# Blocked delta-rule attention before two MoE layers: products taken 22 groups ahead instead of 20, and a queue of transfers put in another order

## The reference

```python
k_n = k / (norm(k) + 1e-06)
for t in range(S):
    y[:, :, t] = einsum('bhd,bhde->bhe', q[:, :, t], state)
    v_old = einsum('bhde,bhd->bhe', state, kt)
    state = state + bt * einsum('bhd,bhe->bhde', kt, vt - v_old)
x = attention_out                    # 3072 tokens x 384
h = x @ w_in;  g = P(h) / (Q(h) + 1e-06);  x = g @ w_out      # first layer
h = x @ w_in;  g = relu(h) ** 2;           out = g @ w_out    # second layer
```

## Time and profile before

| what | us |
|---|---|
| median of three runs (1150.89 to 1154.31) | 1152.41 |
| the profiled execution | 1150.53 |
| its span, first to last instruction | 1148.8 |
| attention: start_z(0) at, last matmul at | 53.1, 339 |
| first matmul of the MoE layers at | 345.1 |

### The profile page before, as it was taken

How to read it: one execution, slowest core, us unless ns; L and a number is a source line. 1 busy time by engine, 2 the same in 40 slices (tenths; PEclk the granted TensorE clock), 3 DMA queues, 4 the chain that set the end, 5 groups by cost and what they waited for, 6 DMA issues and landing times.

```text
span 1148.8 us, 18205 instructions
## 1 busy us (share of the span) xinstructions
PE 1101.6 (96%) x6352; PEld 950.1 (83%) x6352; DVE 674.8 (59%) x1110; ACT 656.2 (57%) x1315; POOL 509.5 (44%) x634
## 2 busy tenths in 40 slices
PE   8798989999878999999999999899999999999998
PEld 6598989999876878888888888788888888888886
DVE  6984445533228988888887878865343333434332
ACT  5665656744448968787777878745333333333332
POOL 5186884877006887777777877600000000000000
PEclk9998989999997999999999999999999999999999
DMA  9937676663504101010100103150010101010000
GB/s 192 205 68 183 125 153 142 112 127 75 152 22 151 42 1 55 1 55 1 56 1 1 56 1 111 42 151 29 20 36 1 55 1 55 1 55 1 1 29 28
DMA packets 173627, 74.42 MB, mean 65 GB/s; under 512 B 135968, under 2 KB 161696, under 8 KB 172576
## 3 DMA queue, kind: packets, MB, share of 16 engines
q1 hardware_dynamic: 163936, 68.54, 24.6%
q10 hardware_dynamic: 9600, 4.72, 1.6%
HBM read 52.27 MB, written 20.71 MB: 64 GB/s over the span
## 4 chain that ended last, share of the span: by engine, by line
PE 64%; DVE 4%; ACT 1%; issue 1%; ACTq 0%
PE ps_y L1118 11%; PE ps_y L1120 11%; PE ps_y L1119 11%; PE ps_h L1103 11%; PE ps_h L1104 11%; PE ps_h L1105 11%; DVE w_out_lo L1240 1%; DVE g_hi L1267 1%; DVE cubic L1252 1%; DVE w_in_lo L1237 0%; DVE g_lo L1282 0%; DVE ps_h L1274 0%; DVE ps_h L1258 0%; ACT w_in_hi L1141 0%; DVE x_lo L1246 0%
## 5 line engine op out<-in xcount | busy, mean ns | idle before, releaser
L1103 PE MATMUL ps_h<-x_hi,w_in_lo 128*128 128x512 f32 x576 | 226.7, 394 | 14.6 <-DVE g_lo L1282 5.9
L1104 PE MATMUL ps_h<-x_lo,w_in_hi 128*128 128x512 f32 x576 | 226.1, 392 | 0.0
L1105 PE MATMUL ps_h<-x_hi,w_in_hi 128*128 128x512 f32 x576 | 225.8, 392 | 0.0
L1118 PE MATMUL ps_y<-g_hi,w_out_lo 128*128 128x512 f32 x576 | 224.5, 390 | 0.1
L1119 PE MATMUL ps_y<-g_lo,w_out_hi 128*128 128x512 f32 x576 | 224.3, 389 | 0.0
L1120 PE MATMUL ps_y<-g_hi,w_out_hi 128*128 128x512 f32 x576 | 224.2, 389 | 0.0
L1293 DVE TENSOR_TENSOR q<-h_sq 128x512 f32<-128x512 f32 x96 | 66.3, 691 | 135.7 <-ACT h_sq L1182 134.1
L1189 ACT ACTIVATE g_hi<-q 128x512 fp32r<-128x512 f32 x96 | 60.7, 633 | 141.8 <-PE ps_y L1120 137.3
L1103 PEld LDWEIGHTS ps_h<-x_hi,w_in_lo 128*128 128x128 f32 x576 | 109.2, 190 | 39.1 <-issue 9.3
L1346 POOL TENSOR_SCALAR den_part<-h_sq,b_abs 128x512 f32<-128x512 f32 x96 | 72.2, 752 | 135.0 <-ACT h_sq L1155 135.0
L1353 POOL TENSOR_TENSOR q<-den_part,b_h 128x512 f32<-128x512 f32 x96 | 124.7, 1299 | 8.2 <-POOL den_part L1346 0.2
(11 more groups left out here) (102 smaller groups left out, 1985.2 us busy)
## 6 DMA issues: line engine op xcount, KB each, us to landing
kq<-kq_in SPq DMA_DIRECT2D x10, 768.0 KB, 5.2
shared<-w_in SPq DMA_DIRECT2D x32, 192.0 KB, 4.2
shared<-w_out SPq DMA_DIRECT2D x32, 192.0 KB, 4.8
vkp<-k_in SPq DMA_DIRECT2D x12, 384.0 KB, 5.7
vkp<-v_in SPq DMA_DIRECT2D x12, 384.0 KB, 6.7
iq<-kq_in SPq DMA_DIRECT2D x12, 384.0 KB, 4.9
x_first<-y_t ACTq DMA_DIRECT2D x24, 192.0 KB, 2.7
shared<-x_first SPq DMA_DIRECT2D x6, 768.0 KB, 6.0
```

What stands on the lines that cost most here:

```text
L1103: pe.matmul(bank(n), lo, x_hi[:, slot, k, :], start=(k == 0), stop=False)
L1104: pe.matmul(bank(n), hi, x_lo[:, slot, k, :], start=False, stop=False)
L1105: mm = pe.matmul(bank(n), hi, x_hi[:, slot, k, :], start=False, stop=(k == KT - 1))
L1118: pe.matmul(ps_y[m][:, :], lo, g_hi[:, d, :], start=(f == 0), stop=False)
```

## The change

The steps with two groups of products are 2 to 8 instead of 2 to 6, so that LEAD is 22 instead of 20, and all 48 groups' products are made by step 25 instead of 27. What goes by that distance moves with it: the stores of N (`step_of_quad`), the loads of `kq`, the steps of the norms. Groups 27 and 29 are taken out by DVE (`mid_group`). On SP, `load_blocks(r)` stands right behind the `store_n` that completes its round, `load_cross` stands ahead of `store_inverse` and of `load_inverse`, and `INV_OUT` asks for the stores of rounds 2 to 5 one or two steps earlier. The masks of groups 8 to 15 are done by DVE, one in each of the steps 8 to 15, and POOL goes from one round to the next. `scale_v` is done two steps later.

```diff
-    TWICE = (2, 6)
+    TWICE = (2, 8)
     LEAD = UPFRONT + TWICE[1] - TWICE[0]
...
-    INV_OUT = (None, 6, 14, 21, 28, 36)
+    INV_OUT = (None, 6, 13, 20, 27, 34)
...
     def step_of_quad(h):
 
-        return {4: 4, 5: 5}[h] if h <= 5 else 4 * h - 16
+        return {4: 4, 5: 5, 6: 7}[h] if h <= 6 else 4 * h + 4 - LEAD
...
         def square_step(h):
-            return 2 * h - 9 if h < 7 else 4 * h - 22
+            return 2 * h - 9 if h < 8 else 4 * h - 24
...
                 for h in range(6, QUADS):
-                    if n == ({6: 4, 7: 6}[h] if h < 8 else 4 * h - 24):
+                    if n == (2 * h - 8 if h < 9 else 4 * h - 26):
                         load_kq(h)
                 for h in range(4, QUADS):
                     if n == step_of_quad(h):
                         store_n(h)
+                for r in range(2, ROUNDS):
+                    if n == step_of_quad(2 * r + 1):
+                        load_blocks(r)
+                for h in range(2, QUADS):
+                    if n == max(4 * h - 3, INV_OUT[h // 2]):
+                        load_cross(h)
                 for r in range(1, ROUNDS):
                     if n == INV_OUT[r]:
                         store_inverse(r)
                 for h in range(2, QUADS):
                     if n == max(4 * h - 3, INV_OUT[h // 2]):
                         load_inverse(h)
-                        load_cross(h)
-                for r in range(2, ROUNDS):
-                    if n == max(8 * r - 12, 6):
-                        load_blocks(r)
...
             pool.wait_ge(placed_by_dve, 2)
-            invert(1)
-            for g in range(FIRST, UPFRONT):
-                mask_products(g)
-            for r in range(2, ROUNDS):
+            for r in range(1, ROUNDS):
                 invert(r)
...
-                if n < FIRST:
+                if n < UPFRONT:
                     pe.wait_ge(p_masked, n + 1)
-                elif n < UPFRONT:
-                    pe.wait_ge(p_by_pool, n - FIRST + 1)
...
-                if n < FIRST:
+                if n < UPFRONT:
                     mask_products(n)
...
                 for h in range(2, QUADS):
-                    if n == (1 if h == 2 else 4 * h - 7):
+                    if n == (1 if h == 2 else 4 * h - 5):
                         scale_v(h)
```

More of the change, by code:

```diff
@@ L147, in build_attention @@
         p_masked = sem("p_masked")
-        p_by_pool = sem("p_by_pool")
         p_ready = sem("p_ready")
@@ L392, in scale_first_v @@
                                    ALU.mult).then_inc(v_by_pool, 1)
[L394 to L398, removed]
             pool.memset(neg_cross[:, :, :], 0.0).then_inc(const_ready, 1)
```

## The result

The changed kernel takes 1140.93 us (median of four runs, 1139.22 to 1141.11), the kernel before 1151.74 in the same comparison (four runs, 1150.89 to 1154.31): a ratio of 0.9899, with a 95% interval from 0.988 to 0.9918, 10.8 us faster. The forecast was 1138.3 and the range 1131.5 to 1144: the result is inside the range, 2.6 us above the number.

The account below looks back on a forecast made before the run. PE, busy for 96% of the span, was taken as the bound, with 20.5 us of stalls to win. Gains of 8.2 + 4.9 + 1.0 = 14.1 us off 1152.4 gave 1138.3 us, range 1131.5 to 1144.

Parts of the forecast that it names:

- The stalls at 16 and 40: PE's waits ahead of steps 16 and 40 were to go wholly, winning 8.2 and 4.9 us.
- The chain given for them: Blocks asked at once, no masks on POOL: its inversions start near 98, 138, 180 and 224 us.
- The masks: Eight mask operations on DVE in steps 8 to 15 cost nothing; without cover 5.7 us.
- The stall at step 8: Losses around step 8 were to be 6.4 us, against 7.4 us before.
- g: The gain at step 8: 1.0 us, with ends of 5.1 and -4.7.
- the wait in step 7: ACT waits 3.8 us for load_kq(7), so PE stalls 3.1 us in step 7, plus 1.7 for the clock.
- the keys of quad 8: load_kq(8) lands near 118.3 us; ACT waits 2.0 us in step 9 and PE loses 1.6.
- I take 99.5, since half a megabyte does stand ahead: Landing time in us taken for load_kq(7), asked behind load_blocks(2) at about 93.5.
- Hidden; at most 0.5 us: At step 8, inverses stored by about 102 and loaded by 106.6 us, before PE is ready at 108.1.
- The first rival: Both loads of kq come in time, PE does not wait in steps 7 to 9: 20.5 us won, 1131.9; chance 0.15.
- 13.1 + g: The attention's total gain: 8.2 us at step 16, 4.9 at step 40, and g at step 8; 14.1 us.

Follow-up runs that it names:

- b1: The kernel before with only load_blocks moved, right behind the store_n that completes its round; 1145.67 us, ratio 0.9972.
- a5: The changed kernel with load_blocks back in its old steps, behind load_inverse; 1146.52 us, ratio 0.9976.
- c1: a2 with load_cross(2) moved to step 5 and load_blocks(2) moved behind store_inverse(1); 1130.43 us, ratio 0.9845.
- d2: c1's queue order and the blocks at once, but products 20 groups ahead as in the kernel before; 1132.64 us, ratio 0.9862.
- a4: The changed kernel with the masks of groups 8 to 15 back on POOL; 1139.08 us, ratio 0.9911.
- b2: The kernel before with only the masks of groups 8 to 15 moved to DVE; 1152.02 us, ratio 1.002.
- a1: The changed kernel with load_kq(7) asked one step earlier, ahead of store_n(5); 1138.73 us, ratio 0.9916.
- a3: The changed kernel with load_cross back behind load_inverse; 1140.74 us, ratio 0.9939.
- d1: The changed kernel with only load_cross(2) moved to step 5 and load_blocks(2) moved behind store_inverse(1); 1133.50 us, ratio 0.9871.
- a2: a1 with load_kq(8) also asked ahead of store_n(6) and load_v(4) one step later; 1137.23 us, ratio 0.9903.

## Why the prediction was right, and where its sum was off

**The stalls at 16 and 40** (8.2 + 4.9 us) were to go wholly, and did. The chain given for them held within 4 us: POOL's starts were forecast for 98, 138, 180 and 224 and came at 99.14, 138.43, 181.85 and 227.94. What it did not see is how the parts share the work. The blocks asked at once take away most of stall 16 and make the one at 8 worse (b1); the rest of the change, with the blocks left in place, halves both later stalls (a5). Which part weighs more stays open: by the medians of kernels beside each other b1 is worth 3.3 us and a5 3.4, of 10.8 and 9.9 for both, and by the stalls of their profiles 3.0 and 7.7, of 11.8. But with the queue in c1's order the distance of 22 groups is worth just 1.6 us of the attention (d2 against c1), and d2, without it, is 17.5 us below the kernel before beside it. So most of what can be won here lies in when the loads and stores are asked.

**The masks** were put at nothing. Neither a4 nor b2 shows a cost or a gain, within the 4 to 5 us that their intervals leave.

**The stall at step 8** is the term that was mis-sized: g = +1.0, measured -1.3 (8.7 lost against 7.4). The mechanism of the wait in step 7 was the forecast one, ACT waiting for `kq` in front of `take_z_first(7)`, and a1 shows it by taking that wait away. The sizes: the keys took 7.7 us to land, not 6.0, so ACT waited 5.6, not 3.8, and PE stood for 4.8, not 3.1; the clock then took 2.65, not 1.7; the keys of quad 8 cost 1.3, not 1.6. The last is partly luck: those keys landed at 121.4, not 118.3, and ACT waited the forecast 2 us only because PE was 3 us late as well. The step that failed is "I take 99.5, since half a megabyte does stand ahead". The prediction had the better value beside it, with the whole 2.2 us of the earlier trace rows for 512 KB added to 5.2: a landing at 100.9 and a PE stall of 4.5 us, and measured were 101.6 and 4.8. Over the five profiles in which the blocks stand right ahead of these keys they took 7.0 to 8.4 us, and 5.2 to 5.8 in the eight others. The Trainium skill (DMA: Bandwidth & Descriptors, section Queues, rings and completion order) says that on each DMA engine descriptors are consumed in the order of the ring; these landings agree.

**"Hidden; at most 0.5 us"**, of the inverses, came out for the wrong reason. Their store was put at 102 and landed at 104.9, and their loads were all there at 108.7, after the 108.1 at which PE was forecast to be ready; it was hidden because PE came only at 111.09. That was luck: one error was covered by another. The first rival, with both loads of keys in time and all 20.5 us won (1131.9), rested on the same error: with the keys in time a1 still loses 6.7 us at step 8, and what it takes to win all of it is c1, at 1130.4.

Of the 13.1 + g the attention shows 11.8, and the medians 10.8; the last 1 us lies within the scatter of the layers. Had g been sized at -1.3, the sum would have been 1152.4 - 11.8 = 1140.6. The number came closer than the sum deserved: for the profiled execution it gave 1136.4, and 1141.11 was measured, 4.7 more, of which 2.3 are g and 2.0 the layers. The 1.9 us by which the median had stood above the profiled execution, taken along in the forecast, were not there in the changed kernel (1140.93 and 1141.11).

**What stays open.** Why the asking of `store_inverse(1)` lasted 4.19 us was not tried by itself. The 512 KB of blocks alone do not do it: in b1, with blocks and keys just ahead, it lasted 0.34, and in a3 0.69. In the six profiles in which cross blocks and queries stand right ahead of it, it lasted 1.5 to 5.2, in a5 (2.02) without any blocks. And b2's attention is 5 us shorter than before's, from lesser stalls at 16 and 40, but its profiled execution (1146.94) was the fastest of its ten, 5.1 us below their median: the attention of one profile tells of that execution, and for a kernel with stalls it can lie that far from the typical one.

## What to carry to other kernels

A transfer that is asked earlier makes all that stand behind it in its queue late: for every one that it is moved past, name who waits for it and how much slack it has, and charge all the bytes ahead at the rate that the trace shows for them. A store that a chain of waits hangs on wants an empty queue, so move what can go early far ahead of it and what can go late behind it. And before you price the removal of a wait, look for the next thing that would be late at the same place: here the wait for keys covered a wait of nearly the same length for inverses. Taking away the first alone won 2 us, and taking away both 8 to 10.

## What the runs showed of the hardware

Asking is not always short. The one instruction of `store_inverse(1)` took SP 0.34 us in before, in c1 and in d1, 1.53 in a2, 4.19 in the changed kernel and 5.17 in its second run, and in that time SP asks for nothing else. The bytes under way do not decide it alone: in b1 1.25 MB of blocks and keys had been asked in the 2.3 us before and not landed, and it took 0.34. The landing of the same 512 KB went from 2.9 to 7.8 us, and that of the 768 KB of keys from 5.2 to 7.7.

What stands behind a transfer seems to cost as well. The 512 KB of `load_blocks(2)` landed 3.5 to 3.7 us after the asking in a1 and a2, where the cross blocks follow, and 5.2 to 6.3 in the changed kernel (both profiles), a3, a4 and b1, where 768 KB of keys follow 0.4 us later. In all of them it stands right behind the stores that it waits for. No run was made for this alone.

The cost of the clock after a stall does not follow its length. PE of the kernel before was idle for 2.98 us ahead of step 40 and lost 1.72 us there to the lower clock; b1 was idle for 2.97 and lost 3.25 (8.15 - 4.90, granted clock 0.59). Before step 16 b2 was idle for 4.44 us and lost 1.70, where before lost 3.3 after 4.77. Here are the two steps of b2:

```profile
149.28:159.69 10.41, 5.97 (x63) 5.78 (x61) 7.27 (x17) 5.41 (x17) 8.92 (x20) 1.00 0.78 169
159.69:167.19 7.50, 7.50 (x61) 7.50 (x62) 1.34 (x2) 2.41 (x6) 6.64 (x12) 0.78 1.15 216
```

In these pairs one stall lost near 1.7 us and the other near twice that; the idle times in step 7 that lasted 3.6 to 5.4 us lost 1.9 to 2.7. Idle times of 1.3 to 1.9 us at the end of step 39 cost next to nothing at the clock (d2 and b2), and so did 3.14 us in step 9 of a5 (granted clock 1.00). But 1.92 us in step 17 of a5 did cost something: its 9.59 us ran at a granted clock of 0.82, part of them at 1.2 instead of 2.4 GHz. The rows do not say what decides.

This fits the spread from execution to execution, though no run was made for it. Of the ten executions of b2, with three stalls, the fastest (1146.94 us) had a mean granted clock of 0.985 and the slowest (1158.25) one of 0.973. The kernel before, with three stalls as well, ran from 1144.6 to 1155.0 us over 44 executions, and c1, with none, from 1129.6 to 1131.5 over four.
